# Linear attention and two MoE layers on one core: another order of the first batch's attention

## The chip, the cores and the metric

One NeuronCore of a Trainium2 chip runs the whole program in one launch. The metric is the device time of that core in microseconds (us); lower is better.

## The reference

```python
def _attn_ref(q, k, v):                       # 4 batches, 8 heads, 576 rows, 64 columns
    q_s = q - np.max(q, axis=-1, keepdims=True)
    q_s = np.exp(q_s)
    q_s = q_s / (np.sum(q_s, axis=-1, keepdims=True) + 1e-09)
    k_s = k - np.max(k, axis=2, keepdims=True)
    k_s = np.exp(k_s)
    k_s = k_s / (np.sum(k_s, axis=2, keepdims=True) + 1e-09)
    kv = np.einsum('bhsd,bhse->bhde', k_s, v)
    return np.einsum('bhsd,bhde->bhse', q_s, kv)

def _moe_ref(x, w_in, w_out, s, b):           # x [2304, 512], w_in [512, 2048], w_out [2048, 512]
    r = np.maximum(x @ w_in, 0.0)
    return (s * (r * r) + b) @ w_out

def _moe2_ref(x, w_in, w_out):
    h = x @ w_in
    return (h * np.tanh(softplus(h))) @ w_out
```

The reference lays the attention's result out as x [2304, 512] and sends it through `_moe_ref` and then `_moe2_ref`. All is float32.

## The kernel before

Each matrix product of the two layers is made of three products of a high and a low part (`win_hi`, `win_lo`, `xs_hi`, `xs_lo`, ...). Tokens are taken in five tiles (four of 512, one of 256). In layer 1 `tile_a` alternates `up` (L790, x times w_in) and `down_a` (L804), and the attention of the next batch is woven into the tile before it. Layer 2 (`tile_b`, L790 and L818) has no attention in it.

Only the attention of the first batch, the **head**, stands in front of the first `up` product. It consists of four units `Unit(0, p)`, of two heads each, 96 partitions by 768 columns. Each engine has its own written order and waits on semaphores:

- SP issues the loads: q of the four units (L218), k of the four (L209), the first quarter of w_in (L234), v in eight halves (L229), two scalars, q and k of unit (1, 0), and then, after a wait for `qsub_done` and `ksub_done`, the first quarter of w_out (L242); then v of (1, 0), which waits for `kv_done`, and the other quarters.
- VectorE takes the row maxima of q (`q_max`, L510) and the column maxima of k within a partition (`k_max`, L505), later the row sums of exp(q) (`q_sum`, `q_eps`, `q_inv`), `k_shift` (L524, k less its column maximum), the low part of the weights (`lo_part`, L592), and `kv_norm` (L544 to L551).
- GpSimd builds the identity `ident` (L297, L299), subtracts the row maxima from q (`q_shift0`, L310), takes the maximum over the partitions (`column_max`, L306) and scales q by the inverse sums (`q_scale0`, L314).
- ScalarE takes the exponentials (`q_exp` L332, `k_exp` L336), moves the transposed q out of PSUM (`take_qT`, L341) and makes the high parts (`win_hi_part` L348, `split_hi` L367, `wout_hi_part` L353).
- TensorE multiplies `ident` by itself 20 times into a bank that nobody reads (L832), then for each unit k by v (`kv_product`, L757), q transposed in two halves (`q_transpose`, L769) and q by kv (`x_product`, L778). The second halves and `x_product` wait for `kv_norm`.

A float32 product stands as two MATMUL records in the trace. Before the first `column_max`, and again before `q_scale0`, the assembled GpSimd program has one ISA instruction that changes its code (MODIFY_POOL_CONFIG in the trace).

Of the kernel before, what the change touches and what calls it, by code (L numbers as in the profile page):

```python
# [8 lines left out]
ALU = mybir.AluOpType  # L9
# [3 lines left out]
P = 128  # L13
TILE = 512
XPASS = 3
LAG_A, LAG_B = 3, 4
HA, HB = 2, 4
WARM_UP = 20
EPS = 1e-9
EXP_CAP = math.exp(20.0)  # L20

# [1 line left out]
def linear_attention_moe_kernel(nc, q, k, v, w_in1, w_out1, s, b, w_in2, w_out2, out):  # L23
# [6 lines left out]
    NP = H // PAIR  # L30
    J = 6
    SP = S // J
# [5 lines left out]
    NG = 4  # L38
# [12 lines left out]
    with ExitStack() as ctx:  # L51
# [48 lines left out]
        s_col, _ = place("s_col", [P, 1])  # L100
        b_col, _ = place("b_col", [P, 1])
        two, _ = place("two", [P, 1])
        assert at[0] <= nc.sbuf_usable_end, at[0]

        Y = [ctx.enter_context(nc.psum_tensor(f"Y{i}", [P, TILE], F32)) for i in range(4)]
# [39 lines left out]
        def per_row(a, n):  # L145
            return a[0:SP, n.p, :].rearrange("s (h j) -> s h j", h=PAIR).unsqueeze(3).to_broadcast([SP, PAIR, J, D])
# [6 lines left out]
        wout_in = [sem(f"wout_in{i}") for i in range(NG)]  # L153
        sb_in = sem("sb_in")
        ident_ready = sem("ident_ready")
        kv_zero = sem("kv_zero")
        ones_ready = sem("ones_ready")
        two_ready = sem("two_ready")
# [46 lines left out]
        @block.sync  # L205
        def _(sp):
            def load_k(n):
                if n.first:
                    sp.dma_start(n.k_raw, k_u[n.u]).then_inc(n.k_in, 16)  # L209
                else:  # L210
                    if not n.fresh:
                        sp.wait_ge(kv_done, n.u)
                    for h in range(PAIR):
                        sp.dma_start(n.k_raw[:, h], k_u[n.u, :, h]).then_inc(n.k_in, 16)

            def load_q(n):
                if n.first:
                    sp.dma_start(n.q_raw, q_u[n.u]).then_inc(n.q_in, 16)  # L218
                else:
                    if not n.fresh:  # L220
                        sp.wait_ge(qT_done[1], n.u)
                    for h in range(PAIR):
                        sp.dma_start(n.q_raw[:, h], q_u[n.u, :, h]).then_inc(n.q_in, 16)

            def load_v(n):
                if not n.first:
                    sp.wait_ge(kv_done, n.u)
                for h in range(PAIR):
                    sp.dma_start(n.v[:, h, :, 0:D], v_u[n.u, :, h]).then_inc(n.v_in, 16)  # L229

            def load_win(layer, i):
                if layer:
                    sp.wait_ge(h_ready, FC * (TILES - 1) + GF * (i + 1))
                sp.dma_start(win_raw[:, :, i * GF * P:(i + 1) * GF * P],  # L234
                             w_in_d[layer][:, :, i * GF * P:(i + 1) * GF * P]).then_inc(win_in[i], 16)

            def load_wout(layer, i):
                if layer and i < NG - 1:
                    sp.wait_ge(g_used, (FC - 1) * (TILES - 1) + GF * (i + 1))
                elif layer:  # L240
                    sp.wait_ge(y_ready, KC * TILES)
                sp.dma_start(wout_raw[:, i * GF:(i + 1) * GF, :],  # L242
                             w_out_d[layer][:, i * GF:(i + 1) * GF, :]).then_inc(wout_in[i], 16)

            def load_unit(n):
                load_q(n)
                load_k(n)
                load_v(n)

            for p in range(NP):  # L250
                load_q(Unit(0, p))
            for p in range(NP):
                load_k(Unit(0, p))
            load_win(0, 0)
            for p in range(NP):
                load_v(Unit(0, p))
            sp.dma_start(s_col[:], s.rearrange("(a n) -> a n", a=1).to_broadcast([P, 1])).then_inc(sb_in, 16)
            sp.dma_start(b_col[:], b.rearrange("(a n) -> a n", a=1).to_broadcast([P, 1])).then_inc(sb_in, 16)
            load_q(Unit(1, 0))
            load_k(Unit(1, 0))  # L260
            sp.wait_ge(qsub_done, NP)
            sp.wait_ge(ksub_done, NP)
            load_wout(0, 0)
            load_v(Unit(1, 0))
            for i in range(1, NG):
                load_win(0, i)
                load_wout(0, i)
            with sp.Fori(0, NEXTRA - 1) as t:
                for p in range(1, NP):
                    load_unit(Unit(t + 1, p))  # L270
                load_unit(Unit(t + 2, 0))
            for p in range(1, NP):
                load_unit(Unit(NEXTRA, p))
            for i in range(NG):
                load_win(1, i)
                load_wout(1, i)

            def store(pos, src, w):
                before = 2 * TILES + y_before(pos) // 2 if isinstance(pos, int) else 2 * TILES + 2 * pos - 1
                for i in range(w // P):  # L280
                    sp.wait_ge(y_taken_dve if i % 2 else y_taken_act, before + i // 2 + 1)
                    rows = out[bass.ds(TILE * src + i * P, P), :]
                    if w == TILE:
                        sp.dma_start(rows, xy_tile(i, src, TILE)).then_inc(stored, 16)
                    else:
                        sp.dma_start(rows.rearrange("r (a n) -> r a n", n=LAST), last_rows(i)).then_inc(stored, 16)

            for pos in (0, 1):
                store(pos, B_ORDER[pos], width(B_ORDER[pos]))
            with sp.Fori(2, TILES) as t:  # L290
                store(t, t - 1, TILE)
            sp.wait_ge(stored, 16 * (N // P))


        @block.gpsimd
        def _(pool):
            nc.gpsimd.memset(ident[:], 0.0).then_inc(ident_ready, 1)  # L297
            pool.wait_ge(ident_ready, 1)
            nc.gpsimd.affine_select(out=ident[:], in_=ident[:], compare_op=ALU.not_equal, fill=1.0, base=0,  # L299
                                    pattern=[[-1, P]], channel_multiplier=1).then_inc(ident_ready, 1)  # L300

            def column_max(n):
                pool.wait_ge(kmax_done, n.u + 1)
                if n.b > 0:
                    pool.wait_ge(ksub_done, n.u)
                nc.gpsimd.partition_all_reduce(n.kcol, n.kmax, SP, bass.bass_isa.ReduceOp.max).then_inc(kcol_done, 1)  # L306

            def q_shift0(n):
                pool.wait_ge(qmax_done, n.u + 1)
                nc.gpsimd.tensor_tensor(n.qh, n.q_raw, per_row(qmax, n), ALU.subtract).then_inc(qsub_done, 1)  # L310

            def q_scale0(n):
                pool.wait_ge(qinv_done, n.u + 1)
                nc.gpsimd.tensor_tensor(n.qh, n.qh, per_row(qinv, n), ALU.mult).then_inc(qnorm_done, 1)  # L314

            for p in range(NP):
                q_shift0(Unit(0, p))
            for p in range(NP):
                column_max(Unit(0, p))
            for p in range(NP):  # L320
                q_scale0(Unit(0, p))
            for p in range(NP):
                column_max(Unit(1, p))
            for batch in range(2, B):
                for p in range(NP):
                    column_max(Unit(batch, p))

        @block.scalar
        def _(act):
# [57 lines left out]

            for p in range(NP):
                q_exp(Unit(0, p))
            win_hi_part(0, 0)  # L390
            for p in range(NP):
                k_exp(Unit(0, p))
            for p in range(NP):
                take_qT(Unit(0, p), [0])
            for p in range(NP):
# [99 lines left out]
        def _(dve):  # L495
# [97 lines left out]
                                        ALU.subtract).then_inc(win_ready if kind == 'in' else wout_ready, 1)  # L593

            for p in range(NP):
                q_max(Unit(0, p))
            for p in range(NP):
                k_max(Unit(0, p))
            for p in range(NP + 1):
                if p < NP:  # L600
                    q_sum(Unit(0, p))
                if p:
                    q_eps(Unit(0, p - 1))
                    k_shift(Unit(0, p - 1))
                    q_inv(Unit(0, p - 1))
            for p in range(NP):
                kv_norm(Unit(0, p))
                if p == 1:
                    lo_part('in', 0, 0)
            for p in range(NP):  # L610
                take_x(Unit(0, p))
                if p >= 1:
# [137 lines left out]
        def _(pe):  # L750
# [72 lines left out]
                    last.then_inc(g_used, 1)  # L823

            pe.wait_ge(ones_ready, NP)
            pe.wait_ge(ident_ready, 2)
            pe.wait_ge(kv_zero, 1)


            pe.wait_ge(qexp_done, 2)  # L830
            for _ in range(WARM_UP):
                nc.tensor.matmul(Hb[NP - 1][:, 0:P], ident[:], ident[:], start=True, stop=True)  # L832
            kv_product(Unit(0, 0))
            for p in range(1, NP):
                kv_product(Unit(0, p))
                q_transpose(Unit(0, p - 1), [0])
            q_transpose(Unit(0, NP - 1), [0])
            q_transpose(Unit(0, 0), [1])
            for p in range(1, NP):
                q_transpose(Unit(0, p), [1])  # L840
# [67 lines left out]
```

## Time and profile before

| | |
|---|---|
| median of 3 runs | 901.88 us (899.53 to 903.38) |
| profiled execution | 902.98 us, of which the span is 901.2 us |
| TensorE busy | 858.3 us, 95% |
| VectorE busy | 608.8 us, 68% |
| ScalarE busy | 378.5 us, 42% |
| GpSimd busy | 30.5 us, 3% |
| first product of layer 1 starts | 51.70 us after the span's start |

The busy time is how long instructions of an engine ran; a wait is not in it, nor is the loading of code. The span starts with the first record of the profile. "Issue" in the chain of waits is time for which the profile shows no releaser.

### The profile page before, as it was taken

What the parts mean: (1) busy time and instruction counts of PE and PEld (TensorE: products, weight loads), DVE (VectorE), ACT (ScalarE), POOL (GpSimd) and SP (SyncE); (2) the same over time, 40 slices, a digit from 0 to 9 for tenths busy, and PEclk for the clock granted to TensorE, in tenths of its full rate; (3) what the DMA queues carried; (4) which work ended last, traced back from release to release, by engine and by line L of the source; (5) the groups of instructions that cost most, each with busy time, mean ns of one, the idle gap of its engine ahead of it and who ended that gap; (6) DMA issues with size and microseconds to landing.
All of it is one profiled execution on the core that took longest, in us unless ns stands there. A gap on an engine that the chain in (4) does not pass through costs nothing.

```text
span 901.2 us, 11133 instructions
## 1 busy us (share of the span) xinstructions
PE 858.3 (95%) x4136; PEld 720.9 (80%) x4136; DVE 608.8 (68%) x1033; ACT 378.5 (42%) x621; POOL 30.5 (3%) x30
## 2 busy tenths in 40 slices
PE   2689999999999999999999899998999999999998
PEld 2568888888888888888998678897888788878886
DVE  5578875755576554322356889788697879777975
ACT  2245443423343333222356445455454445444543
POOL 2400000100000000000000000000000000000000
PEclk9599999999999999999999999999899999999999
DMA  8281111111101110000144000100000010000001
GB/s 204 76 290 40 40 40 40 40 40 40 40 13 39 39 27 1 1 0 1 47 158 171 0 1 1 47 1 1 24 0 1 1 47 0 0 10 37 0 0 47
DMA packets 60645, 36.15 MB, mean 40 GB/s; under 512 B 48320, under 2 KB 50368, under 8 KB 60608
## 3 DMA queue, kind: packets, MB, share of 16 engines
q1 hardware_dynamic: 60608, 35.66, 13.8%
q8 instruction: 23, 0.38, 0.2%
q14 instruction: 14, 0.11, 0.0%
HBM read 30.93 MB, written 4.72 MB: 40 GB/s over the span
## 4 chain that ended last, share of the span: by engine, by line
PE 80%; DVE 9%; ACT 5%; issue 4%; POOL 1%; DVEq 0%; ACTq 0%; POOLq 0%
PE H L790 38%; PE Y L804 20%; PE Y L818 16%; PE H L757 2%; PE H L778 1%; ACT t L452 1%; DVE g L696 1%; DVE t L668 1%; ACT t L454 1%; DVE wout_lo L592 1%; DVE t L673 1%; ACT wout_hi L353 1%; PE H L769 1%; DVE t L678 1%; DVE win_lo L592 1%
## 5 line engine op out<-in xcount | busy, mean ns | idle before, releaser
L790 PE MATMUL H<-xs_hi,win_hi 128*128 128x512 f32 (+1 forms) x640 | 240.4, 376 | 7.6 <-DVE g_raw L691 3.3
L790 PE MATMUL H<-xs_lo,win_hi 128*128 128x512 f32 (+1 forms) x640 | 236.7, 370 | 0.0
L790 PE MATMUL H<-xs_hi,win_lo 128*128 128x512 f32 (+1 forms) x640 | 236.6, 370 | 0.0
L818 PE MATMUL Y<-wout_hi,g 128*128 128x512 f32 x576 | 190.5, 394 | 5.5 <-DVE g L696 5.5
L804 PE MATMUL Y<-g,wout_hi 128*128 128x512 f32 (+1 forms) x640 | 183.2, 371 | 0.7 <-DVE g L576 0.7
L790 PEld LDWEIGHTS H<-xs_hi,win_hi 128*128 128x128 f32 x640 | 121.4, 190 | 30.0 <-DVE g_raw L691 4.0
L790 PEld LDWEIGHTS H<-xs_hi,win_lo 128*128 128x128 f32 x640 | 121.3, 190 | 20.6
L790 PEld LDWEIGHTS H<-xs_lo,win_hi 128*128 128x128 f32 x640 | 121.3, 190 | 20.5
L818 PEld LDWEIGHTS Y<-wout_hi,g 128*128 128x128 f32 x576 | 108.8, 189 | 31.1 <-DVE g L696 8.7
L804 PEld LDWEIGHTS Y<-g,wout_hi 128*128 128x128 f32 x640 | 115.2, 189 | 20.0 <-DVE g L576 0.9
L571 DVE SCALAR_TENSOR_TENSOR g_raw<-g_raw,s_col 128x512 f32<-128x512 f32 (+1 forms) x80 | 55.5, 694 | 95.9 <-ACT g_raw L374 95.6
L804 PE MATMUL Y<-g,wout_lo 128*128 128x512 f32 (+1 forms) x320 | 117.8, 368 | 0.0
L452 ACT ACTIVATE t<-t,two 128x512 f32<-128x512 f32 (+1 forms) x80 | 54.6, 682 | 142.1 <-DVE t L668 142.1
L374 ACT ACTIVATE g_raw<-H 128x512 f32<-128x512 f32 (+1 forms) x80 | 44.0, 550 | 165.1 <-PE Y L804 154.2
L818 PE MATMUL Y<-wout_lo,g 128*128 128x512 f32 x288 | 113.0, 392 | 0.0
L576 DVE SCALAR_TENSOR_TENSOR g<-g_raw,b_col,g 128x512 fp32r<-128x512 f32 (+1 forms) x80 | 55.9, 698 | 60.6 <-ACT g L378 60.6
L378 ACT ACTIVATE g<-g_raw,b_col 128x512 fp32r<-128x512 f32 (+1 forms) x80 | 54.2, 678 | 91.4 <-DVE g_raw L571 91.4
L804 PEld LDWEIGHTS Y<-g,wout_lo 128*128 128x128 f32 x320 | 60.3, 189 | 10.2
L818 PEld LDWEIGHTS Y<-wout_lo,g 128*128 128x128 f32 x288 | 54.5, 189 | 10.7
L673 DVE TENSOR_TENSOR t<-t,t 128x512 f32<-128x512 f32 (+1 forms) x80 | 51.1, 639 | 16.7 <-ACT t L454 8.9
L447 ACT ACTIVATE t<-H 128x512 f32<-128x512 f32 (+1 forms) x80 | 43.6, 544 | 39.2 <-PE H L790 39.2
L663 DVE TENSOR_SCALAR t<-t 128x512 f32<-128x512 f32 (+1 forms) x80 | 31.6, 395 | 34.4 <-ACT t L447 34.4
(71 smaller groups left out, 818.5 us busy)
## 6 DMA issues: line engine op xcount, KB each, us to landing
win_raw<-in_moe_w_in_dram SPq DMA_DIRECT2D x8, 1024.0 KB, 7.5
wout_raw<-in_moe_w_out_dram SPq DMA_DIRECT2D x8, 1024.0 KB, 5.1
g_flat<-in_v_dram SPq DMA_DIRECT2D x32, 144.0 KB, 3.3
out_dram<-xy SPq DMA_DIRECT2D x18, 256.0 KB, 2.1
qbuf<-in_q_dram SPq DMA_DIRECT2D x24, 144.0 KB, 2.9
kbuf<-in_k_dram SPq DMA_DIRECT2D x24, 144.0 KB, 3.1
raw<-in_q_dram SPq DMA_DIRECT2D x4, 288.0 KB, 4.6
raw<-in_k_dram SPq DMA_DIRECT2D x4, 288.0 KB, 7.7
```

The source lines that it names most:

```text
L374: nc.scalar.activation(g_raw[:, f % LAG_A, 1, 0:w], Hb[f % HA][:, 0:w], ACT.Relu).then_inc(ha_taken, 1)
L378: nc.scalar.activation(g[:, f % LAG_A, 0, 0:w], g_raw[:, f % LAG_A, 1, 0:w], ACT.Identity, bias=b_col[:]).then_inc(ghi_done, 1)
L447: nc.scalar.activation(t1[:, f % 2, 0:w], Hb[f % HB][:, 0:w], ACT.Exp).then_inc(e_done, 1)
L452: nc.scalar.activation(t2[:, f % 2, 0:w], t1[:, f % 2, 0:w], ACT.Ln, bias=two[:]).then_inc(ln_done, 1)
L571: nc.vector.scalar_tensor_tensor(r, r, s_col[:], r, ALU.mult, ALU.mult).then_inc(sq_done, 1)
L576: nc.vector.scalar_tensor_tensor(g[:, f % LAG_A, 1, 0:w], g_raw[:, f % LAG_A, 1, 0:w], b_col[:], g[:, f % LAG_A, 0, 0:w].bitcast(F32), ALU ...
L592: nc.vector.tensor_tensor(lo, raw, hi.bitcast(F32), ALU.subtract).then_inc(win_ready if kind == 'in' else wout_ready, 1)
L663: nc.vector.tensor_scalar_min(t, t, EXP_CAP).then_inc(min_done, 1)
L673: nc.vector.tensor_tensor(t, t, t2[:, f % 2, 0:w], ALU.mult).then_inc(c_done, 1)
L790: last = nc.tensor.matmul(Hb[f % banks][:, 0:w], a[:, i, cols], m[:, i, 0:w], start=(i == 0 and n == 0), stop=(i == KC - 1 and n == XPASS ...
L804: last = nc.tensor.matmul(Y[i][:, 0:w], a[:, f, cols], g[:, f % LAG_A, m, 0:w], start=(f == 0 and n == 0), stop=(f == FC - 1 and n == XPAS ...
L818: last = nc.tensor.matmul(Y[i][:, :], g[:, f % LAG_B, a, rows], m[:, f, :], start=(f == 0 and n == 0), stop=(f == FC - 1 and n == XPASS - 1))
```

## The change

The order of the head changes on every engine. Loads: k, then q of unit 0, then q and v in turn, then the first quarters of w_in and of w_out with no wait, q and k of (1, 0), the second quarters, and only then v of (1, 0), which waits. GpSimd starts with a maximum over the partitions of a column of zeros (`idle_column_max(1)`), does the real ones, then the identity, then `q_scale0`, then an idle maximum again. `q_shift0` is gone from GpSimd; VectorE does `q_shift` for the first batch too. TensorE does 18 products of the zeroed `kv` tile (128x512) in place of 20 products of `ident` (128x128), from the start and not after `qexp_done`; all four `kv_product` come ahead of the transposes. `kv` is zeroed by VectorE at the start in both kernels.

```diff
-WARM_UP = 20
+WARM_UP = 18
@@ SP
+            for p in range(NP):
+                load_k(Unit(0, p))
+            load_q(Unit(0, 0))
+            for p in range(1, NP):
                 load_q(Unit(0, p))
-            for p in range(NP):
-                load_k(Unit(0, p))
+                load_v(Unit(0, p - 1))
+            load_v(Unit(0, NP - 1))
             load_win(0, 0)
-            for p in range(NP):
-                load_v(Unit(0, p))
...
+            load_wout(0, 0)
             load_q(Unit(1, 0))
             load_k(Unit(1, 0))
-            sp.wait_ge(qsub_done, NP)
-            sp.wait_ge(ksub_done, NP)
-            load_wout(0, 0)
+            load_win(0, 1)
+            load_wout(0, 1)
             load_v(Unit(1, 0))
-            for i in range(1, NG):
+            for i in range(2, NG):
@@ GpSimd
+            def idle_column_max(n):
+                nc.gpsimd.memset(spare[:, 0:1], 0.0).then_inc(idle_max, 1)
+                pool.wait_ge(idle_max, 2 * n - 1)
+                nc.gpsimd.partition_all_reduce(spare[0:SP, 1:2], spare[0:SP, 0:1], SP,
+                                               bass.bass_isa.ReduceOp.max).then_inc(idle_max, 1)
...
-            for p in range(NP):
-                q_shift0(Unit(0, p))
+            idle_column_max(1)
             for p in range(NP):
                 column_max(Unit(0, p))
+            make_ident()
             for p in range(NP):
                 q_scale0(Unit(0, p))
+            idle_column_max(2)
@@ ScalarE
             for p in range(NP):
                 q_exp(Unit(0, p))
+                k_exp(Unit(0, p))
             win_hi_part(0, 0)
-            for p in range(NP):
-                k_exp(Unit(0, p))
@@ VectorE
             for p in range(NP):
+                k_max(Unit(0, p))
+            for p in range(NP):
                 q_max(Unit(0, p))
-            for p in range(NP):
-                k_max(Unit(0, p))
+                q_shift(Unit(0, p))
+                k_shift(Unit(0, p))
             for p in range(NP + 1):
                 if p < NP:
                     q_sum(Unit(0, p))
                 if p:
                     q_eps(Unit(0, p - 1))
-                    k_shift(Unit(0, p - 1))
                     q_inv(Unit(0, p - 1))
+            lo_part('in', 0, 0)
             for p in range(NP):
                 kv_norm(Unit(0, p))
-                if p == 1:
-                    lo_part('in', 0, 0)
@@ TensorE
             pe.wait_ge(ones_ready, NP)
-            pe.wait_ge(ident_ready, 2)
             pe.wait_ge(kv_zero, 1)
-            pe.wait_ge(qexp_done, 2)
             for _ in range(WARM_UP):
-                nc.tensor.matmul(Hb[NP - 1][:, 0:P], ident[:], ident[:], start=True, stop=True)
-            kv_product(Unit(0, 0))
-            for p in range(1, NP):
-                kv_product(Unit(0, p))
-                q_transpose(Unit(0, p - 1), [0])
-            q_transpose(Unit(0, NP - 1), [0])
+                nc.tensor.matmul(Hb[NP - 1][:, 0:TILE], kv[:, 0, :], kv[:].rearrange("p a n -> p (a n)"),
+                                 start=True, stop=True)
+            for p in range(NP):
+                kv_product(Unit(0, p))
+            pe.wait_ge(ident_ready, 2)
+            for p in range(NP):
+                q_transpose(Unit(0, p), [0])
```

On GpSimd, the head in the order of issue before:

```order
L299 ISA [waits ident_ready]
L299 AFFINE_SELECT ident<-ident 128x128
L310 TENSOR_TENSOR xy<-raw_53,qmax 96x2x6x64 [waits qmax_done] x4
L306 ISA
L306 ISA xs_raw<-xs_raw 96x128 [waits kmax_done] x4
L314 ISA
L314 TENSOR_TENSOR xy<-xy,qinv 96x2x6x64 [waits qinv_done] x4
```

and on GpSimd in the changed kernel, whose lines from here on have numbers 3 to 7 higher (L316 is the `column_max`, L309 the idle one):

```order
L307 MEMSET spare 128x1
L309 ISA
L309 ISA spare<-spare 96x1 [waits idle_max]
L316 ISA xs_raw<-xs_raw 96x128 [waits kmax_done] x4
L301 MEMSET ident 128x128
L303 AFFINE_SELECT ident<-ident 128x128 [waits ident_ready]
L320 ISA
L320 TENSOR_TENSOR xy<-xy,qinv 96x2x6x64 [waits qinv_done] x4
```

Three code changes became two in the head, the four subtractions left, and one ISA instruction of the code change now stands in front of everything.

On VectorE, the sums of q before, with `k_shift` between them (`L524`):

```order
L505 TENSOR_REDUCE xs_raw<-raw_53 96x128 [waits k_in0_3]
L528 TENSOR_REDUCE qsum<-xy 96x12 [waits qexp_done] x2
L533 TENSOR_SCALAR qeps<-qsum 96x12 [waits qsum_done]
L524 TENSOR_TENSOR xy<-raw_53,xs_raw 96x2x6x64 [waits kcol_done]
L537 RECIPROCAL qinv<-qeps 96x12 [waits qeps_done]
```

and on VectorE behind the four `k_max` in the changed kernel (one unit, and the first sums; L521 is the subtraction that GpSimd did):

```order
L511 TENSOR_REDUCE xs_raw<-raw_53 96x128 [waits k_in0_3]
L516 TENSOR_REDUCE qmax<-raw_53 96x12 [waits q_in0_0]
L521 TENSOR_TENSOR xy<-raw_53,qmax 96x2x6x64 [waits qmax_done]
L530 TENSOR_TENSOR xy<-raw_53,xs_raw 96x2x6x64 [waits kcol_done]
L534 TENSOR_REDUCE qsum<-xy 96x12 [waits qexp_done] x2
L539 TENSOR_SCALAR qeps<-qsum 96x12 [waits qsum_done]
L543 RECIPROCAL qinv<-qeps 96x12 [waits qeps_done]
```

`k_shift` moved ahead of all sums, and each unit's `q_shift` stands in front of its `k_shift`.

## Rows read from the trace of the kernel before

**Rows 1.** The page: granted TensorE clock, 40 slices of the span

```profile
PEclk9599999999999999999999999999899999999999
```

**Rows 2.** Busy time by stretch: PE, PEld, DVE, ACT, POOL, clock, DMA

```profile
0.00:51.70 51.70, 26.27 (x129) 23.93 (x129) 27.65 (x58) 15.66 (x20) 16.98 (x18) 0.77 0.62 163
51.70:901.20 849.50, 831.99 (x4010) 696.94 (x4008) 581.16 (x976) 362.82 (x601) 13.54 (x12) 0.99 0.11 33
```

**Rows 3.** Timeline of GpSimd: start, duration, line, count, [idle before, releaser]

```profile
0.73 0.20 POOL L297 MEMSET ident<- 128x128 f32 x1 [0.29 <-POOLq L897]
11.00 0.28 POOL L299 TENSOR_SCALAR_AFFINE_SELECT ident<-ident 128x128 f32<-128x128 f32 x1 [10.07 <-issue]
11.28 5.76 POOL L310 TENSOR_TENSOR xy<-raw,qmax 96x768 f32<-96x768 f32 x4
23.41 3.19 POOL L306 PARTITION_ALL_REDUCE xs_raw<-xs_raw  x4 [6.37 <-issue]
33.60 7.36 POOL L314 TENSOR_TENSOR xy<-xy,qinv 96x768 f32<-96x768 f32 x4 [7.00 <-issue]
```

**Rows 4.** Timeline of VectorE, first 12 us

```profile
3.92 1.99 DVE L510 TENSOR_REDUCE qmax<-raw 96x12 f32<-96x768 f32 x2 [2.44 <-DMA raw<-in_q_dram]
7.20 0.95 DVE L510 TENSOR_REDUCE qmax<-raw 96x12 f32<-96x768 f32 x1 [1.30 <-DMA raw<-in_q_dram]
8.35 0.95 DVE L510 TENSOR_REDUCE qmax<-raw 96x12 f32<-96x768 f32 x1 [0.20 <-DMA raw<-in_q_dram]
9.46 5.59 DVE L505 TENSOR_REDUCE xs_raw<-raw 96x128 f32<-96x768 f32 x4 [0.16 <-DMA raw<-in_k_dram]
```

**Rows 5.** Timeline of VectorE, 24 to 45 us

```profile
24.16 1.18 DVE L524 TENSOR_TENSOR xy<-raw,xs_raw 96x768 f32<-96x768 f32 x1 [7.09 <-POOL xs_raw L306]
...
25.40 0.89 DVE L528 TENSOR_REDUCE qsum<-xy 96x12 f32<-96x768 f32 x1
...
26.28 0.94 DVE L524 TENSOR_TENSOR xy<-raw,xs_raw 96x768 f32<-96x768 f32 x1
27.15 0.21 DVE L537 RECIPROCAL qinv<-qeps 96x12 f32<-96x12 f32 x1
27.29 0.89 DVE L528 TENSOR_REDUCE qsum<-xy 96x12 f32<-96x768 f32 x1
...
33.04 2.29 DVE L592 TENSOR_TENSOR win_lo<-win_raw,win_hi 128x2048 fp32r<-128x2048 f32 x1
...
43.28 0.33 DVE L544 TENSOR_SCALAR ksum<-Y 64x1 f32<-64x1 f32 x2 [1.99 <-PE Y L757]
...
43.84 0.58 DVE L551 TENSOR_SCALAR kv<-Y,kinv 64x64 f32<-64x64 f32 x2
```

**Rows 6.** Timeline of VectorE, 57 to 61 us: the second batch

```profile
57.74 0.94 DVE L510 TENSOR_REDUCE qmax<-qbuf 96x12 f32<-96x768 f32 x1
58.71 0.95 DVE L515 TENSOR_TENSOR qbuf<-qbuf,qmax 96x768 f32<-96x768 f32 x1
59.59 1.51 DVE L505 TENSOR_REDUCE kmax<-kbuf 96x128 f32<-96x768 f32 x1
```

**Rows 7.** TensorE by stretch: length, busy (MATMUL records), granted clock, DMA

```profile
15.20:18.30 3.10, 3.10 (x14) 1.00 1.00 152
18.30:21.40 3.10, 3.08 (x28) 1.00 0.63 133
21.40:25.10 3.70, 0.00 (x0) 1.00 0.83 159
25.10:49.00 23.90, 17.39 (x75) 0.50 0.30 92
```

**Rows 8.** Timeline of TensorE

```profile
26.27 5.57 PE L757 MATMUL Y<-g_flat,xy 96*128 96x130 f32 x24 [4.90 <-ACT xy L336]
...
43.04 1.17 PE L769 MATMUL H<-ident,xy 96*128 96x96 f32 x6
...
45.62 1.30 PE L778 MATMUL Y<-xy,kv 128*128 128x288 f32 x2 [0.46 <-ACT xy L341]
...
51.70 0.61 PE L790 MATMUL H<-xs_hi,win_hi 128*128 128x512 f32 x1
```

**Rows 9.** One line's durations, TensorE: min/median/max ns

```profile
L832 PE MATMUL H<-ident x40: 274/275/553, 15.2 to 21.1; 128*128 128x128 f32 x40
```

**Rows 10.** DMA issues before 60 us: KB each, median us to landing

```profile
g_flat<-in_v_dram SPq DMA_DIRECT2D x12, 144.0 KB, 3.7
```

More of the change, by code:

```diff
@@ L102, in linear_attention_moe_kernel @@
         two, _ = place("two", [P, 1])
+        spare, _ = place("spare", [P, 2])
         assert at[0] <= nc.sbuf_usable_end, at[0]
@@ L155, in linear_attention_moe_kernel @@
         ident_ready = sem("ident_ready")
+        idle_max = sem("idle_max")
         kv_zero = sem("kv_zero")
@@ L296, in _, with make_ident @@
         def _(pool):
[L297 to L300, printed above, removed]
+            def make_ident():
+                nc.gpsimd.memset(ident[:], 0.0).then_inc(ident_ready, 1)
+                pool.wait_ge(ident_ready, 1)
+                nc.gpsimd.affine_select(out=ident[:], in_=ident[:], compare_op=ALU.not_equal, fill=1.0, base=0,
+                                        pattern=[[-1, P]], channel_multiplier=1).then_inc(ident_ready, 1)
+            def idle_column_max(n):
[3 more added lines that the diff above has]
+                                               bass.bass_isa.ReduceOp.max).then_inc(idle_max, 1)
             def column_max(n):
@@ L306, in column_max @@
                 nc.gpsimd.partition_all_reduce(n.kcol, n.kmax, SP, bass.bass_isa.ReduceOp.max).then_inc(kcol_done, 1)
-            def q_shift0(n):
-                pool.wait_ge(qmax_done, n.u + 1)
-                nc.gpsimd.tensor_tensor(n.qh, n.q_raw, per_row(qmax, n), ALU.subtract).then_inc(qsub_done, 1)
             def q_scale0(n):
@@ L825, in _ @@
             pe.wait_ge(ones_ready, NP)
-            pe.wait_ge(ident_ready, 2)
-            pe.wait_ge(kv_zero, 1)
-            pe.wait_ge(qexp_done, 2)
-            for _ in range(WARM_UP):
-                nc.tensor.matmul(Hb[NP - 1][:, 0:P], ident[:], ident[:], start=True, stop=True)
-            kv_product(Unit(0, 0))
-            for p in range(1, NP):
-                kv_product(Unit(0, p))
-                q_transpose(Unit(0, p - 1), [0])
-            q_transpose(Unit(0, NP - 1), [0])
+            pe.wait_ge(kv_zero, 1)
+            for _ in range(WARM_UP):
+                nc.tensor.matmul(Hb[NP - 1][:, 0:TILE], kv[:, 0, :], kv[:].rearrange("p a n -> p (a n)"),
+                                 start=True, stop=True)
+            for p in range(NP):
+                kv_product(Unit(0, p))
+            pe.wait_ge(ident_ready, 2)
+            for p in range(NP):
+                q_transpose(Unit(0, p), [0])
             q_transpose(Unit(0, 0), [1])
```

## The prediction

> **What bounds the kernel now.** I read the page first, for the shares and the clock by slices [rows 1], then busy time by stretch [rows 2], then the chain of waits and the timelines of the head, engine by engine. From 51.70 us to the end TensorE is busy 831.99 of 849.50 us: nothing that the change touches can gain there. The first 51.70 us are another matter: TensorE's useful work there is small and every engine is idle for about half of it. So the question is at what time the first `up` product can start, and the rest of the program is moved by as much.
>
> What sets that time is seen on GpSimd [rows 3]. Its first real instruction starts at 11.00 although the memset before it ended at 0.93: 10.07 us of idle time with no releaser, behind the ISA instruction that loads code. Then come four subtractions (5.76 us, to 17.04), 6.37 us without a releaser (the code for the maxima), four maxima (3.19 us, to 26.60), 7.00 us again (the code for the multiplications), and four multiplications from 33.60 to 40.96. VectorE waits 7.09 us for the first maximum [rows 5], and TensorE's transposes wait for the multiplications. From the x product of unit 0 at 45.62 to the first `up` at 51.70 there are 6.08 us [rows 8]. The first half of this path is code loading and order, not arithmetic.
>
> **The change, step by step.** I write the new head as a schedule, in us from the span's start. For neighbouring VectorE instructions I count start to start, since the shown durations overlap a little.
>
> *Loads and k maxima.* k now has the places in the queue that q had. Those landed by 3.92, before the second maximum, at 7.20 and 8.35, and the fifth load at 9.46 [rows 4]. A `k_max` takes 5.59 / 4 = 1.40. So they run 3.92 to 6.7, 7.2 to 8.6 and 8.6 to 10.0. The fifth load, q of unit 0, is there by then.
>
> *First code load.* Instruction 1 of GpSimd still waits for its code until 11.00 (taken from the row of the same place, 10.07 of idle time). The idle maximum and four real ones take 3.19 / 4 = 0.80 each. A waiting k_shift started 24.16 - 23.41 = 0.75 after its maximum started. So the first real result is there at 11.0 + 0.80 + 0.75 = 12.55 and the last at 15.0. The lower bound for the load is the 6.37 of the next one: it would free VectorE from waiting from 11.9 to 12.6 and give 0.7 more. The Trainium skill (GPSIMD Engine Reference, the section on how an instruction is dispatched, step on wrapper-ucode) gives about 6 us for the first call of freshly loaded code. By that figure the 0.7 would be had; the row at the start has 10.07, and I go by the row. The upper bound is a rival below.
>
> *VectorE.* `q_max` to `q_shift` is 58.71 - 57.74 = 0.97, `q_shift` to the next 59.59 - 58.71 = 0.88 [rows 6], `k_shift` to the next 27.15 - 26.28 = 0.87 [rows 5]: 2.72 for a unit. The first `q_max` and `q_shift` end at 11.9, the first `k_shift` runs 12.6 to 13.5, and three more units end at 13.5 + 8.2 = 21.7. This adds four subtractions to VectorE (3.5 us), which lie on the path; they remove 5.76 us from GpSimd. The sums: between 25.40 and 27.29 stand one sum, one eps, one k_shift and one inverse, so without the k_shift a unit takes 1.89 - 0.87 = 1.02; four end at 25.8, the first `q_inv` at about 23.6. `lo_part` follows to about 28.1 (2.29, [rows 5]), then four `kv_norm` of 43.84 + 0.58 - 43.28 = 1.14 each, to 32.7.
>
> *TensorE.* 18 products are 36 MATMUL records of four times the columns. Before, 14 records took 3.10 us and then 28 took 3.10 us [rows 7]: 0.22 and 0.11 each, the 1.2 GHz and the 2.4 GHz level (the clock column prints 1.00 for both stretches, its first recorded event is the rise at 18.3). Four times that is 0.89 and 0.44. From 1.9 us on, with 3.1 us at the low level as before, that is 3.5 records and 32.5 records of 0.44: the end is near 1.9 + 3.1 + 14.4 = 19.4. The first exponential of k is ready at 14.4, the last at 22.6, so the warm-up delays only the first kv products. At the high level one takes half of 5.57 / 2 = 2.79 [rows 8], 1.4; the last ends at 24.0, behind the last exponential. The 1.95 us between the first and the second pair of transposes that kv products filled before is gone. Should they run at 1.2 GHz, the four end at 19.4 + 11.1 = 30.5, still ahead of the last `kv_norm` by its order, and cost under 1 us. Products were at half clock from 25.1 to 49.0 [rows 7], 3.7 us after the last busy instruction; I assume the same for the x products and so no gain from the clock.
>
> *Second code load and multiplications.* The maxima end at 15.0, the identity takes 0.5. Taking 7.00 for the load of the same code [rows 3], GpSimd is ready at 22.5, before the first inverse at 23.6: the load is now hidden. At the bound of 10.07 it would be ready at 25.6 and cost 1.5. A multiplication takes 1.44 (as L310: 5.76 / 4). The first of them took 7.36 - 3 x 1.44 = 3.04 while `lo_part` ran beside it from 33.04 to 35.33 [rows 3, 5]: 1.6 more. The same meets the second and third now, since `lo_part` runs 25.8 to 28.1. So they end at 25.0, 26.8 to 28.5, 30.0 and 31.4. The transpose of unit 3 starts at 31.4 and ends at 31.9, ScalarE moves two blocks (0.65 each), and the first x product starts at about 33.3. The last `kv_norm` at 32.7 is in time. Add 6.08: the first `up` starts at **39.4**.
>
> *Two engines, one memory.* The first `k_shift` took 1.18 while maxima ran, the second 0.94 [rows 5]. Four such tensor_tensor instructions of VectorE now run beside maxima: 4 x 0.24 = 1.0. The Trainium skill (GPSIMD Engine Reference, key points) says that GpSimd shares its memory interfaces with VectorE and contends with instructions of two inputs. By the rule the reverse can happen too, a maximum that waits for VectorE. The rows show this for the multiplication under `lo_part`. For the maxima a stretch of up to 0.95 each would not matter past the first, since VectorE asks for one every 2.7 us. With the 1.0 the first `up` is at 40.4.
>
> *Weight loads.* w_out's first quarter loses a wait and both second quarters come early. They follow everything that the head needs, so they cost nothing unless GpSimd's code load is slowed by traffic; that bound is the 10.07 above. `up` did not wait for weights before, so nothing is gained either. v of unit (1, 0) waits for all four kv products; behind it stand only the third and fourth quarters, needed tens of us later. The second idle maximum costs nothing: the first `column_max` of the second batch had 20 us of slack.
>
> **The sum.** 51.7 - 40.4 = 11.3 us less, 902.98 - 11.3 = 891.7 against the profiled execution. That execution was 1.1 above the median of the runs, 901.88, so against the median I predict **890.6**. A measurement of this kernel can tell about 0.5%, 4.5 us, from no change.
>
> **The rivals.**
> 1. *The first 10 us are not the code load.* If something else ends at 11.00 (the engine's start-up), the code for the maximum comes on top with 6.37 us. Then the first maximum is done at 18.9, `k_shift` of unit 0 starts 6.4 later, and all behind it: 11.3 - 6.4 = 4.9 gained, 897.0. For it: the loads of 6.37 and 7.00 are alike and the first is 3 to 4 us longer. Against: the first row also stands behind just one code instruction, and 3.7 us are not enough for a second load of 6. Chance 0.14, split between faster 0.08 and same 0.06.
> 2. *q arrives late.* v halves of small packets now stand between the loads of q. Of 144 KB halves, each takes 3.7 us to land [rows 10], and q of unit 3 has four of them ahead. I put its landing at 9.5 + 1.1 x 3 + 4 x 0.85 = 16.2, needed at 18.9. If each half costs twice that, it lands at 19.6, and with win_in late too the loss is 1 to 5 us: about 893 to 896. Chance 0.07, faster 0.04 and same 0.03.
> 3. *The warm-up holds TensorE up (slower).* The queue of TensorE is in order, so kv products stand behind 36 records. If the 512-wide records take four times the shown median of 0.275 [rows 9], or the clock does not rise for zeros and each takes over 0.89, they end late: from their end to the last first-half transpose are 4 x 2.79 + 3 x 0.49 = 12.6, and that transpose started at 43.7 before (the second half of the row at 43.04). The point of no gain is an end at 31.1, or 0.81 a record. At 0.275 x 4 = 1.10 they end at 41.5, and the time is 901.9 + 10.4 = 912. Against it: the record's duration is latency, and 28 records in 3.10 us show the rate. Chance 0.04.
>
> The forecast has the remaining 0.75. Faster is 0.75 + 0.08 + 0.04 = 0.87, same 0.09, slower 0.04. The range goes from 888 (no contention, a short first load and 1 us of scatter) to 898 (rival 1 and 1 us of scatter).
>
> **What would show it.** Right: the idle maximum starts near 11, VectorE waits under 1 us for the first real one, the multiplications start when the first inverse is ready, the first `up` starts near 40, and the rest of the span is 849 to 850 as now. Wrong: an idle gap on GpSimd of over 14 us at the start (rival 1), a VectorE wait on the loads of q (rival 2), kv products that wait for nothing but the warm-up past 25 (rival 3), or a stretch behind the first `up` that is longer than 849.5 by over 2 us.

## The result and the profile after

The changed kernel takes **891.5 us** (median of 4 runs, 890.38 to 892.73) against 901.92 (median of 4, 899.53 to 903.38): ratio 0.9889, 95% interval 0.9871 to 0.9908. It is faster by 1.1%. The forecast was 890.6, range 888 to 898. The profiled execution took 890.38, its span is 888.6 us.

The granted clock of the page after, to be read against [rows 1]: the second slice has 7 where it had 5, since the stretch at 1.2 GHz is shorter.

```profile
PEclk9799999999999999999999999999999999999999
```

Busy time by stretch, cut where the first `up` product starts (columns as in [rows 2]):

```profile
0.00:40.10 40.10, 33.75 (x123) 20.48 (x124) 32.36 (x62) 15.72 (x20) 12.97 (x18) 0.87 1.04 272
40.10:888.60 848.50, 831.39 (x4010) 697.05 (x4008) 581.16 (x977) 362.93 (x601) 13.60 (x12) 0.99 0.10 30
```

The head went from 51.70 to 40.1 us. The rest took 849.50 us and now takes 848.50, with TensorE busy 831.99 and 831.39; a difference of 1 us is less than what lies between the runs of one kernel (890.38 to 892.73), and the end of the experiments shows what it goes with. So nearly all of the gain is the head, as forecast. GpSimd's timeline after answers to [rows 3]:

```profile
0.73 0.10 POOL L307 MEMSET spare<- 128x1 f32 x1 [0.29 <-POOLq L900]
0.95 0.36 POOL L309 PARTITION_ALL_REDUCE spare<-spare  x1
5.34 0.70 POOL L316 PARTITION_ALL_REDUCE xs_raw<-xs_raw  x1 [4.02 <-DVE xs_raw L511]
...
9.47 0.70 POOL L316 PARTITION_ALL_REDUCE xs_raw<-xs_raw  x1 [0.69 <-DVE xs_raw L511]
...
22.50 1.47 POOL L320 TENSOR_TENSOR xy<-xy,qinv 96x768 f32<-96x768 f32 x1 [11.12 <-DVE qinv L543]
24.34 1.47 POOL L320 TENSOR_TENSOR xy<-xy,qinv 96x768 f32<-96x768 f32 x1 [0.37 <-DVE qinv L543]
26.18 5.10 POOL L320 TENSOR_TENSOR xy<-xy,qinv 96x768 f32<-96x768 f32 x2 [0.37 <-DVE qinv L543]
```

Here is the surprise. The idle maximum starts at 0.95, behind an ISA instruction that changes the code, and the first real one at 5.34, as soon as VectorE delivers (L511 is `k_max`, L316 `column_max`, L320 `q_scale0`). The 10.07 us with no releaser at the head of [rows 3] are not late or hidden, they are gone. The multiplications start with their data, 22.50.

VectorE's timeline after, which has no gap from the first `k_max` to the last `kv_norm` (L516 is `q_max`, L530 `k_shift`, L534 `q_sum`, L539 `q_eps`, L598 `lo_part`):

```profile
3.79 5.59 DVE L511 TENSOR_REDUCE xs_raw<-raw 96x128 f32<-96x768 f32 x4 [2.31 <-DMA raw<-in_k_dram]
9.30 0.94 DVE L516 TENSOR_REDUCE qmax<-raw 96x12 f32<-96x768 f32 x1
...
11.15 1.04 DVE L530 TENSOR_TENSOR xy<-raw,xs_raw 96x768 f32<-96x768 f32 x1
...
20.28 1.80 DVE L534 TENSOR_REDUCE qsum<-xy 96x12 f32<-96x768 f32 x2
22.00 0.16 DVE L539 TENSOR_SCALAR qeps<-qsum 96x12 f32<-96x12 f32 x1
...
23.15 0.86 DVE L539 TENSOR_SCALAR qeps<-qsum 96x12 f32<-96x12 f32 x1
...
25.00 0.85 DVE L539 TENSOR_SCALAR qeps<-qsum 96x12 f32<-96x12 f32 x1
...
26.30 2.22 DVE L598 TENSOR_TENSOR win_lo<-win_raw,win_hi 128x2048 fp32r<-128x2048 f32 x1
```

The second and third `q_eps`, with 12 elements a partition, take 0.86 and 0.85 where the first takes 0.16. Each stands beside a multiplication of GpSimd (22.50 to 23.97, 24.34 to 25.81) and ends about when it ends. And the last two multiplications take 5.10 together, not 2.94: `lo_part` runs beside them. TensorE after (L834 are the products of zeros, L763 is `kv_product`, L775 `q_transpose`, L784 `x_product`, L796 `up`):

```profile
1.54 18.58 PE L834 MATMUL H<-kv 128*128 128x512 f32 x36 [1.54 <-DVE g_flat L505]
19.96 5.53 PE L763 MATMUL Y<-g_flat,xy 96*128 96x130 f32 x48
...
31.34 0.74 PE L775 MATMUL H<-ident,xy 96*128 96x96 f32 x3 [0.69 <-POOL xy L320]
...
33.45 1.30 PE L784 MATMUL Y<-xy,kv 128*128 128x288 f32 x2 [0.41 <-ACT xy L348]
...
40.13 0.61 PE L796 MATMUL H<-xs_hi,win_hi 128*128 128x512 f32 x1
```

The products of zeros end at 20.0, the kv products run at twice their old pace (48 records in 5.53 us; before 24 in 5.57, [rows 8]) and end at 25.5. Unit 0's transposes wait for them from 24.0 to 25.3, off the path: the path goes through the last multiplication.

The head can be followed further in three pieces. The last multiplication ended at 40.96 and ends at 31.28, 9.7 us earlier. From there to the first x product it was 4.7 us and is 2.2, so 2.5 us come from TensorE's part. In the kernel before, TensorE was inside the `kv_product` of unit 3 when the last multiplication ended:

```profile
40.38 2.86 PE L757 MATMUL Y<-g_flat,xy 96*128 96x130 f32 x12
```

Its transposes began at 43.04 [rows 8]; now all `kv_product` are done before. No run puts the old order of TensorE back, so these 2.5 us are read from the traces and not tested. From the first x product to the first `up` are 6.68 us, against 6.08.

### The profile page after: what moved, and what is told of

The parts are those of the page before. It is cut to its first block, busy times and chain, and to the rows that moved or that the text cites. A ratio compares the mean times of both kernels' runs of the same rounds, so it can differ in the third digit from the quotient of the medians.

```text
span 888.6 us, 11126 instructions
## 1 busy us (share of the span) xinstructions
PE 865.1 (97%) x4132; PEld 717.5 (81%) x4132; DVE 613.5 (69%) x1037; ACT 378.7 (43%) x621; POOL 26.6 (3%) x30
## 4 chain that ended last, share of the span: by engine, by line
PE 80%; DVE 11%; ACT 6%; issue 2%; POOL 1%; DMA 0%; DVEq 0%; ACTq 0%
PE H L796 38%; PE Y L810 21%; PE Y L824 17%; PE H L763 2%; PE H L784 2%; ACT t L458 1%; DVE g L702 1%; DVE t L674 1%; ACT t L460 1%; DVE wout_lo L598 1%; DVE t L679 1%; ACT wout_hi L360 1%; DVE t L684 1%; PE H L775 1%; DVE win_lo L598 1%
## 5 line engine op out<-in xcount | busy, mean ns | idle before, releaser
L796 PE MATMUL H<-xs_hi,win_hi 128*128 128x512 f32 (+1 forms) x640 | 240.8, 376 | 7.7 <-DVE g_raw L697 3.3
L796 PE MATMUL H<-xs_hi,win_lo 128*128 128x512 f32 (+1 forms) x640 | 236.8, 370 | 0.0
L796 PE MATMUL H<-xs_lo,win_hi 128*128 128x512 f32 (+1 forms) x640 | 236.7, 370 | 0.0
L796 PEld LDWEIGHTS H<-xs_hi,win_hi 128*128 128x128 f32 x640 | 121.4, 190 | 30.0 <-DVE g_raw L697 4.0
L796 PEld LDWEIGHTS H<-xs_hi,win_lo 128*128 128x128 f32 x640 | 121.3, 190 | 20.8
L796 PEld LDWEIGHTS H<-xs_lo,win_hi 128*128 128x128 f32 x640 | 121.4, 190 | 20.4
```

Source lines behind the costliest of these rows:

```text
L796: last = nc.tensor.matmul(Hb[f % banks][:, 0:w], a[:, i, cols], m[:, i, 0:w], start=(i == 0 and n == 0), stop=(i == KC - 1 and n == XPASS ...
```

## The experiments

I compare the kernels by the start of the first `up` product in their traces, since that is where the change acts; the rest of the span differs between executions by up to 2.5 us, as the end of this section shows. Each such start comes from one execution; two executions of the changed kernel have 40.13 and 39.73. Times are medians; ratios are to the kernel before in the same call.

**Which code GpSimd holds at the start.** In the kernel before, one GpSimd instruction behind everything else:

```diff
+            pool.wait_ge(kcol_done, B * NP)
+            nc.gpsimd.tensor_tensor(kmax1[0:SP, :], kmax1[0:SP, :], kmax1[0:SP, :], ALU.mult)
```

> The kernel before with one small GpSimd multiplication behind the last maximum over partitions (near 350 us), so that GpSimd ends the program with the code of its elementwise instructions. It leaves out nothing. Theory 'kept code' (the code that GpSimd holds at the end of one execution is there at the start of the next, so a program that begins with other code than it ended with pays a load): the identity's select starts near 1.2 us and not at 11.0, the four subtractions follow the q loads (5 to 11 us), and the maxima, waiting for their own code, end 6 to 8 us earlier; first up product 5 to 8 us earlier, near 45. Rival 'first load' (whatever stands first pays about 10 us at the start, unless it is a maximum, whose code comes with the program): select at 11.0 as before, first up at 51.7, time 902.

Measured: 895.74 us, ratio 0.9941 (0.9918 to 0.9964), first `up` at 45.25. GpSimd's timeline:

```profile
1.42 0.30 POOL L299 TENSOR_SCALAR_AFFINE_SELECT ident<-ident 128x128 f32<-128x128 f32 x1 [0.49 <-POOL ident L297]
5.04 5.76 POOL L310 TENSOR_TENSOR xy<-raw,qmax 96x768 f32<-96x768 f32 x4 [3.32 <-DVE qmax L512]
16.88 3.19 POOL L306 PARTITION_ALL_REDUCE xs_raw<-xs_raw  x4 [6.08 <-issue]
27.38 7.06 POOL L314 TENSOR_TENSOR xy<-xy,qinv 96x768 f32<-96x768 f32 x4 [7.30 <-issue]
```

The select, at 11.00 before, starts at 1.42, and the first `up` comes 6.45 us earlier. Nothing in the head was changed; the instruction that changes the code still stands in front of the select. The same multiplication put at the end of the changed kernel must then do harm:

> The changed kernel with the same GpSimd multiplication behind the last maximum. 'Kept code': now the idle maximum of the start has to load its code; it or the first real one starts near 6 to 11 us, VectorE waits up to 2 us for it, the first up product moves from 40.1 to 40 to 43. Rival 'first load': idle maximum at 0.95, first up at 40.1.

Measured: 891.84 us, ratio 0.9899 (0.9855 to 0.9944), first `up` at 40.38.

```profile
8.49 0.38 POOL L309 PARTITION_ALL_REDUCE spare<-spare  x1 [7.66 <-issue]
8.79 3.25 POOL L316 PARTITION_ALL_REDUCE xs_raw<-xs_raw  x4
```

Now the idle maximum waits 7.66 us for its code. VectorE asks for the first result at 11.4, when it is there, so this costs next to nothing: the first `up` is 0.25 later, less than lies between two executions of the changed kernel. Both runs say the same: an execution starts with the code that the last one ended with. The kernel before ends with maxima and starts with a change to the elementwise code, in front of the select; the changed kernel ends and starts with maxima. What the first launch of a program does, or one behind another program, was not measured.

**The first idle maximum.**

```diff
-            idle_column_max(1)
```

> The changed kernel without its first idle maximum: the first real one is the first instruction behind the code change. If code is there at the start ('kept code' or code that comes with the program), or if its load begins at the code instruction and not at the first maximum, nothing moves: first real maximum at 5.3, first up at 40.1. If the idle maximum is what pays, by my prediction's picture, the first maximum starts later than 10 and first up comes 1 to 6 us later.

Measured: 891.36 us, ratio 0.9903 (0.987 to 0.9936), first real maximum at 5.53, first `up` at 40.08. It does nothing that can be seen.

**The products of zeros** (`WARM_UP = 0`).

> The changed kernel without the 18 products of zeros. It leaves out work that nobody reads. My sum: the kv products are not on the path, so at half clock they start at 13 and end by 24; first up moves by under 0.5 us. Rival: without them the clock is low when the first up products run (the kernel before had its rise at 49.0, 2.7 us before the first up), and 1 to 3 us are lost between the first up and the end of the first tile.

Measured: 890.04 us, ratio 0.9887 (0.9848 to 0.9926), first `up` at 39.76. The kv products start at 13.45 and take their time:

```profile
13.45 10.93 PE L763 MATMUL Y<-g_flat,xy 96*128 96x130 f32 x48 [13.45 <-ACT xy L343]
```

At the slow pace, 10.93 us, they end at 24.4, 0.3 us behind the first multiplication (24.1) and long before the last. The rest took 848.0 us, so nothing was lost behind the first `up` either. In this kernel the products of zeros buy nothing.

**Where the low part stands.**

```diff
-            lo_part('in', 0, 0)
             for p in range(NP):
                 kv_norm(Unit(0, p))
+            lo_part('in', 0, 0)
```

> The changed kernel with the first low part of the weights (2.22 us on VectorE, two inputs in memory) behind the four kv_norm and not ahead of them. Theory 'shared port on the path': the third multiplication of GpSimd ran beside it and the last two took 5.10 and not 2.94; so without it they end at about 29.1 and not 31.28, and first up comes at 38.0 to 38.5 and not 40.13, time 889.5. Rival 'VectorE is the bound': the last kv_norm and the low part together end as before at 33.1, the copies of x wait, and first up moves by under 0.5.

Measured: 889.57 us, ratio 0.9854 (0.9825 to 0.9882), first `up` at 37.80, 2.33 earlier.

```profile
26.49 2.90 POOL L320 TENSOR_TENSOR xy<-xy,qinv 96x768 f32<-96x768 f32 x2 [0.36 <-DVE qinv L543]
```

The two multiplications take 2.90, not 5.10: it was `lo_part` that held GpSimd, and the transposes with it. The first x product starts at 31.55 and not 33.45, 1.9 us earlier; the remaining 0.4 us lie between it and the first `up` (6.25 us and not 6.68), where the clock rises sooner.

**The subtraction of q back on GpSimd**, behind the maxima and the identity, with k's exponentials first:

```diff
+            for p in range(NP):
+                q_shift0(Unit(0, p))
             for p in range(NP):
                 q_scale0(Unit(0, p))
...
-                q_shift(Unit(0, p))
-                k_shift(Unit(0, p))
+            for p in range(NP):
+                k_shift(Unit(0, p))
```

> The changed kernel with the subtraction of q's maxima back on GpSimd (behind the maxima, the identity and the code change), k's exponentials ahead of q's on ScalarE. By my prediction's sums the load of 7 to 8 us starts at 11.4, so the subtractions run 18.5 to 24.3, the multiplications from 24.3 to 30 or 31.7 (low part beside them), and first up is at 39 to 41: moving the subtraction to VectorE bought nearly nothing once the maxima come first. Rival: the load was hidden only by the subtractions on VectorE; its cost is back on the path, first up at 44 or later, time 895 or more.

Measured: 895.92 us, ratio 0.9924 (0.9895 to 0.9953), first `up` at 44.19. The expectation of 39 to 41 was wrong.

```profile
17.91 7.22 POOL L320 TENSOR_TENSOR xy<-raw,qmax 96x768 f32<-96x768 f32 x4 [6.83 <-issue]
```

```profile
16.26 6.10 DVE L537 TENSOR_TENSOR xy<-raw,xs_raw 96x768 f32<-96x768 f32 x4
24.00 1.81 DVE L541 TENSOR_REDUCE qsum<-xy 96x12 f32<-96x768 f32 x2 [1.64 <-ACT xy L345]
```

(GpSimd, then VectorE.) The code took 6.83 us as assumed. What I left out is that the subtractions of both engines meet: GpSimd's four take 7.22 (5.76 in [rows 3]) and VectorE's four 6.10 (0.95 each in the changed kernel). They meet because of my order for VectorE: all `q_max` stand ahead of all `k_shift`, and the last two waited for the loads of q:

```profile
15.39 0.95 DVE L523 TENSOR_REDUCE qmax<-raw 96x12 f32<-96x768 f32 x1 [1.67 <-DMA raw<-in_q_dram]
```

So the first `k_shift` started at 16.26, where it started at 11.15. In addition my order for ScalarE put the first exponential of q behind all of k's, and VectorE's sums waited 1.64 us for it; the sums began at 24.0 where they began at 20.28. So the changed kernel is 4.1 us ahead of this one, but part of that is my VectorE order and my ScalarE order. The shares were not tried apart, and what the move of the subtraction alone is worth stays open.

**The loads in the old order** (q, k, w_in, v):

> The changed kernel with the head's loads in the old order: q, k, first quarter of w_in, v. VectorE still begins with k_max, which waits for the fifth load at about 9.4: all of VectorE's chain moves by 9.4 - 3.8 = 5.6 less what can be taken up, first up at 44.5 to 46, time 896 to 897. Rival (k first is not what matters, the GpSimd code is): first up at 40 to 42.

Measured: 895.6 us, ratio 0.9933 (0.9908 to 0.9958), first `up` at 44.83, 4.70 later. The first `k_max` waits for its load until 9.19:

```profile
9.19 2.85 DVE L510 TENSOR_REDUCE xs_raw<-raw 96x128 f32<-96x768 f32 x2 [7.71 <-DMA raw<-in_k_dram]
```

It started 5.4 us later than at 3.79, and all of that reaches the first x product (38.88 and not 33.45). That also shows how completely VectorE's chain holds the path. The first `up` comes only 4.7 later, since from the x product to it are 5.95 us and not 6.68.

**The weight loads as before**, with the wait for `qsub_done` and `ksub_done` and v of (1, 0) ahead of the second quarters:

> The changed kernel with the weight loads as before: w_out's first quarter behind the waits for qsub_done and ksub_done, v of the second batch ahead of the second quarters. My sum says the early weights are worth nothing: first up at 40.1, and the stretch behind it as long as before (848 to 850). Rival: transfers beside the head slow it; then first up comes up to 0.5 us earlier here, or weights come late in the first tile and the stretch is over 1 us longer.

Measured: 891.08 us, ratio 0.9871 (0.9835 to 0.9906), first `up` at 40.53, rest 850.0. The early loads are worth at most 0.4 us in the head, about the spread between two executions of the changed kernel (40.13 and 39.73), and the first `k_max` started 0.30 later here (4.09 and 3.79). The rest is 1.5 us longer than in the changed kernel; since its length goes with stretches of the clock, shown below, I don't put this down to the weights.

**What is best.** The lean kernel leaves out the idle maximum and the products of zeros and has the low part behind `kv_norm`; the changed kernel ran beside it.

> The changed kernel without the first idle maximum, without the 18 products of zeros, and with the first low part behind the four kv_norm. By the runs so far (low part behind: first up at 37.8; no products and no idle maximum: 39.8 to 40.1, so nothing lost) first up comes at 37.5 to 38.2 and the time is 888 to 889, 2 to 3 below the changed kernel of the same call. Rival: the three do not add (the clock falls in the first tile, 2 to 3 us lost behind first up): 890 to 891.

> The changed kernel itself on the same chip as the lean one, as its yardstick: 891.5 (890 to 893), first up at 40.1 to 40.5, ratio to the kernel before 0.988 to 0.989.

Measured: lean 889.73 us, ratio 0.9871 (0.9852 to 0.989), first `up` at 38.38; changed kernel again 891.16, ratio 0.99 (0.9884 to 0.9917), first `up` at 39.73. At the first `up` the gain is 1.35 us here, not 2.33. Two more kernels then looked for the difference:

> The lean kernel with the 18 products of zeros back. In the kernel with the low part moved and the products kept, first up was at 37.80; without products and idle maximum at 38.38, where the x products still ran at 1.2 GHz until 37. 'The products help once the head is short': first up at 37.8 and 888.5 to 889.5, 0.3 to 1 below the lean kernel. Rival: no difference, first up at 38.4.

Measured: 889.04 us, ratio 0.9868 (0.9848 to 0.9889), first `up` at 37.97, which is 0.41 earlier than the lean kernel. The x products of the lean kernel:

```profile
34.98 1.17 PE L783 MATMUL H<-xy,kv 128*128 128x288 f32 x2
35.94 0.69 PE L774 MATMUL Y<-ident,xy 96*128 96x96 f32 x3
36.42 0.89 PE L783 MATMUL Y<-xy,kv 128*128 128x288 f32 x2
37.14 0.65 PE L783 MATMUL H<-xy,kv 128*128 128x288 f32 x2
```

They still ran at the 1.2 GHz level until about 36.5; with the products of zeros the clock rises at about 35.4. But this moment also differs between two executions of one kernel: 38.1 and about 37.0 in the changed one. So the 0.41 us are not shown to be the work of the zeros, and the medians of the two kernels, 889.73 and 889.04, do not tell them apart either.

What the low part is worth shows better ahead of this rise, from the first `k_max` to the first x product:

| kernel | first `k_max` | first x product | between | first `up` |
|---|---|---|---|---|
| changed | 3.79 | 33.45 | 29.66 | 40.13 |
| changed again | 3.98 | 33.63 | 29.65 | 39.73 |
| no products of zeros | 4.00 | 33.58 | 29.58 | 39.76 |
| old loads | 9.19 | 38.88 | 29.69 | 44.83 |
| weights wait | 4.09 | 33.78 | 29.69 | 40.53 |
| low part behind | 4.08 | 31.55 | 27.47 | 37.80 |
| lean | 4.07 | 31.43 | 27.36 | 38.38 |
| lean with zeros | 4.24 | 31.71 | 27.47 | 37.97 |

Moving the low part gives 2.2 us in every one of its kernels. What made it 2.33 once and 1.35 once is when k landed and when the clock rose, not the kernel.

> The lean kernel with zeros, with the multiplication of q by its inverse sums on VectorE for all four units, so that GpSimd does maxima and the identity alone and changes its code nowhere. VectorE gains 4 x 0.87 = 3.5 us and loses the two eps of 0.86 that stood behind a GpSimd multiplication (1.4 back): its low part ends 2.1 us later, at 35.6, first up at 39.5 to 40 and 891. Rival (GpSimd's multiplications, not VectorE, hold the transposes): transposes end 1 to 2 us earlier, first up at 37 to 37.8.

```diff
             for p in range(NP):
-                q_scale0(Unit(0, p))
...
                     q_inv(Unit(0, p - 1))
+                    q_scale(Unit(0, p - 1))
```

Measured: 889.08 us, ratio 0.9873 (0.9855 to 0.9891), first `up` at 39.33, just under the expected 39.5. All `q_eps` take 0.16, none 0.86: the long ones did stand behind GpSimd's multiplication. The head is longer with more work on VectorE, as expected with VectorE as the bound. Yet the time equals that of the kernel above, whose head is 1.36 us shorter.

**The rest of the span** explains that. From first `up` to the end, the profiled executions took 849.5 (before), 848.5 (changed), 848.0 (changed again), 847.8 (the last kernel), 849.3 (lean with zeros) and 850.3 us (lean), at the same instructions. Clock of the lean kernel with zeros and of the last one, from 50 to 60 us (column behind POOL; 1.00 is the 2.4 GHz level):

```profile
50.00:60.00 10.00, 10.00 (x41) 8.22 (x42) 7.61 (x10) 5.44 (x7) 0.00 (x0) 0.70 0.14 31
```

```profile
50.00:60.00 10.00, 8.37 (x45) 6.88 (x46) 8.24 (x11) 5.17 (x10) 0.00 (x0) 1.00 0.14 31
```

TensorE has a pause of 2.8 us that starts about 9 us behind the first `up` in all of them, the kernel before too (it waits there for `g_raw`). In some the clock is at 1.2 GHz for a stretch just behind it, in others not. But this place alone does not settle it, since the kernel before has no such stretch there and still took 849.5. Two others lie near 495 and 620 us (505 and 632 in the kernel before). From 612 to 640 us, the kernel before, the lean one with zeros and the last one:

```profile
612.00:640.00 28.00, 25.03 (x116) 20.15 (x116) 19.03 (x50) 12.63 (x31) 0.00 (x0) 0.88 0.06 19
```

```profile
612.00:640.00 28.00, 24.41 (x106) 19.22 (x105) 20.92 (x41) 13.79 (x27) 0.00 (x0) 1.00 0.06 20
```

```profile
612.00:640.00 28.00, 25.44 (x103) 19.98 (x103) 20.52 (x40) 13.42 (x25) 0.00 (x0) 0.94 0.06 20
```

The slow stretches of the rest, its last microseconds apart, are short ones of about 3 us or long ones of about 7, and the executions of all runs sort by them. With a short one at each of the two late places the rest took 847.8 to 848.0 us. With a long one just behind the pause and none later it took 849.2 to 849.5, and with a short and a long one at the late places 849.5. With all three places slow, one of them long, it took 850.0 to 850.3. The changed kernel's 848.5 has three short ones. What decides where a stretch falls was not settled. They go with differences of 1 to 2.5 us, and below that size the runs here cannot rank the variants.

## Why the prediction was right, and where it was right by luck

The number, 890.6 for 891.5, and the place, the first `up` at 40.4 for 40.13 and an unchanged rest, came out. Of its steps:

- *Loads and k maxima.* Right: `k_max` ran from 3.79 to 9.38, forecast 3.92 to 10.0. The load order is worth 4.7 us at the first `up`, the largest single piece that was undone alone in the changed kernel.
- *First code load.* **Wrong.** I took 10.07 from the row of the same place and its lower bound from the next load, 6.37. The true value is zero, since the code was there from the execution before. The row showed the price of a change from the program's last code to its first, and I read it as the price of being first. Rival 1 erred in the other direction. In the sum it mattered little: by the forecast's own schedule VectorE could use only 0.7 us of it. As a cause it matters: the kernel before gains 6.45 us by this effect alone.
- *Two engines, one memory.* **Misplaced.** The 1.0 us was for four subtractions of VectorE beside maxima. They never met: with the code there from the start the last maximum ended at 10.17, and the first `q_shift` started at 10.28. The first `k_shift` took 1.04 beside the identity's select, all others 0.95. Where they did meet, in the changed kernel with the multiplication at its end (maxima until 12.04), `q_shift` took 1.00 and `k_shift` 1.15, together 0.25 more. What did stretch were the two `q_eps` beside multiplications, 0.7 each, for which I had no term. I had weighed the Trainium skill's rule on this (GPSIMD Engine Reference, key points) for instructions of two inputs. The trace agrees with it for the multiplications beside `lo_part`. A `q_eps` has one input, and no run here shows by what rule it was held.
- *Luck in the sum.* With the 1.0 us in it, the forecast of 40.4 had the last `k_shift` end at 22.7 (measured 20.4), the first multiplication start at 24.6 (22.50), the last one end at 32.4 (31.28) and the first x product start at 34.3 (33.45). The lead of 2.3 us shrank to 1.1 by the two `q_eps` and by `lo_part`, and the x products took another 0.6. The first `up` came within 0.3 us because errors of opposite sign nearly cancelled.
- *lo_part beside the multiplications.* Right as mechanism and in size (2.2 us for the last two, forecast 1.6); the experiment confirms it.
- *TensorE.* Right that it is off the path: the zeros ended at 20.0 (19.4), the kv products at 25.5 (24.0). The 24.0 was a slip of the sum: four products of 1.4 behind 19.4 end at 25.0. The zeros are worth nothing that these runs show. The order of TensorE took 2.5 us off between the last multiplication and the first x product, as the schedule had it (1.9 us for that piece, measured 2.2). Rival 3 did not happen: 36 records took 18.4 us, 0.51 each.
- *Second code load hidden.* Right: the multiplications waited for `q_inv`. Its length can't be seen there; with the subtractions on GpSimd it was 6.83. (At the bound of 10.07 the forecast's own times give a cost of 25.6 - 23.6 = 2.0, not 1.5.)
- *Weight loads at nothing.* Consistent with the run that undid them; up to 0.4 us stays within the spread.
- *x products and the last piece.* 6.68 us for 6.08: the clock rose at about 38.1, 2.0 us before the first `up`, where before it was 2.7, so more of the x products ran at 1.2 GHz. I had assumed equality. In the second execution of the changed kernel it was 6.10.

## What to carry to other kernels

Idle time of GpSimd ahead of its first real instruction may be a change of code from what the previous execution ended with. Begin and end the program with instructions of the same kind, or end it with one cheap instruction of the kind it begins with: in the kernel before that was 6.45 us in the head for one instruction. When the head of a kernel is a chain on VectorE, first give it the data it starts with, then keep its two-input instructions away from GpSimd's, and only then think of TensorE's clock. And to tell variants of 1 us apart, cut the trace into pieces and compare each: here the clock's stretches behind the head are as large as what is sought.

## What the runs showed of the hardware

- GpSimd's code stays from one execution to the next. With the right code kept, the first instruction started at 0.95 to 1.42 us; with the wrong one at 8.49 (maxima) or 11.00 (select). Later changes took 6.1 to 9.7 us, and the traces give no reason for the spread; the idle maximum behind the multiplications paid 6.5 to 9.7 us of it where nobody waited (8.2 in the changed kernel's profile).
- In the changed kernel the select ran behind the maxima without another change of code.
- A VectorE instruction of 12 elements took 0.86 and not 0.16 us beside a GpSimd multiplication, and a GpSimd pair took 5.10 and not 2.90 us beside a 2.2 us VectorE subtraction. Beside maxima on GpSimd a VectorE subtraction took 1.00 to 1.18 and not 0.95, and VectorE's sums beside a multiplication took 0.89, as they did without one in [rows 5].
- Products of zeros bring TensorE to 2.4 GHz: 36 records took 18.4 us, where 36 at 0.89 (an estimate, four times the 0.22 of the low level in [rows 7]) would take 32.
